# An unused tensor of 32 bytes behind the constants of an attention + mixture-of-experts kernel

## The reference, cut to what matters

```python
# q, k, v: (4 batches, 8 heads, 576 positions, 64); window 64
scores = q @ k.T / 8, masked to 0 <= i - j < 64, softmax, @ v   -> x: (2304, 512)
# mixture of experts, E = 8, hidden 1024
noisy = x @ w_gate + log1p(exp(x @ w_noise)) * noise
top2 of noisy per token, softmax over the two
out[token] += weight * (relu(x[token] @ w1[e]) @ w2[e])          # its two experts
# dense layer, hidden 2048
h = x @ w_in;  g = h if h >= 1, 0 if h <= -1, else (h + 1)**2 / 4
return g @ w_out
```

## Time and profile before

| | |
|---|---|
| runs | 1139.37, 1140.97, 1141.70 us; median 1140.97 us |
| profiled execution | 1140.15 us, span 1138.6 us from first to last instruction |
| mean granted TensorE clock | 0.976 of full speed |
| PE busy | 1086.2 us, 95% of the span |
| PEld, DVE, ACT, POOL busy | 928.5, 346.6, 351.7, 355.0 us |
| DMA | 121.96 MB, mean 107 GB/s |
| chain that ended last | PE 81%, DMA 8%, POOL 7% |

### The profile page before, as it was taken

How to read it: one execution, slowest core, us unless ns; L and a number is a source line. 1 busy time by engine, 2 the same in 40 slices (tenths; PEclk the granted TensorE clock), 3 DMA queues, 4 the chain that set the end, 5 groups by cost and what they waited for, 6 DMA issues and landing times.

```text
span 1138.6 us, 19459 instructions
## 1 busy us (share of the span) xinstructions
PE 1086.2 (95%) x6597; PEld 928.5 (82%) x6598; DVE 346.6 (30%) x652; ACT 351.7 (31%) x797; POOL 355.0 (31%) x230
## 2 busy tenths in 40 slices
PE   7999489997699999999999999999999999999998
PEld 5998368886588888888888887889889899898896
DVE  5888621221011221121122112334132242241421
ACT  4676312121121222122222212425234143252441
POOL 3000067434882917345361803750110101101000
PEclk8999689999799999999999999999999999999999
DMA  9896355778353333324141422220110101101000
GB/s 233 222 228 158 121 176 185 229 256 288 96 181 111 120 120 111 111 92 147 53 169 55 140 73 65 91 77 10 55 40 15 55 0 55 46 9 55 8 12 19
DMA packets 68706, 121.96 MB, mean 107 GB/s; under 512 B 25728, under 2 KB 30976, under 8 KB 68160
## 3 DMA queue, kind: packets, MB, share of 16 engines
q0 software_dynamic: 16688, 62.66, 17.1%
q1 hardware_dynamic: 38496, 34.72, 11.0%
q10 hardware_dynamic: 13488, 24.12, 6.5%
HBM read 87.66 MB, written 33.82 MB: 107 GB/s over the span
## 4 chain that ended last, share of the span: by engine, by line
PE 81%; DMA 8%; POOL 7%; issue 2%; DVE 1%; SPq 0%; ACT 0%; POOLq 0%; DVEq 0%
PE bank L1115 6%; PE bank L1114 6%; PE bank L1113 6%; PE bank L1053 6%; PE bank L1051 6%; PE bank L1052 6%; PE bank L1036 5%; PE bank L1038 5%; PE bank L1037 5%; PE bank L1100 5%; PE bank L1099 5%; PE bank L1098 5%; POOL Wl L378 4%; DMA x_sorted<-gath 3%; DMA gath<-x_rows,token_of 3%; PE bank L924 3%
## 5 line engine op out<-in xcount | busy, mean ns | idle before, releaser
L378 POOL TENSOR_TENSOR Wl<-stage,Wh 128x2048 fp32r<-128x2048 f32 x36 | 165.8, 4606 | 3.0
L1098 PE MATMUL bank<-zT_h,Wh 128*128 128x256 f32 x576 | 161.9, 281 | 1.0 <-DVE zT_l L861 1.0
L1099 PE MATMUL bank<-zT_l,Wh 128*128 128x256 f32 x576 | 161.8, 281 | 0.0
L1100 PE MATMUL bank<-zT_h,Wl 128*128 128x256 f32 x576 | 161.7, 281 | 0.0
L1036 PE MATMUL bank<-Wh,xT_h 128*128 x344 | 141.1, 410 | 19.7 <-POOL Wl L378 18.1
L827 DVE COPY y_out<-bank 128x512 f32<-128x512 f32 x43 | 29.7, 691 | 393.1 <-PE bank L1053 393.1
L1038 PE MATMUL bank<-Wh,xT_l 128*128 x344 | 137.4, 399 | 0.0
L1037 PE MATMUL bank<-Wl,xT_h 128*128 x344 | 136.6, 397 | 0.0
L1053 PE MATMUL bank<-Wh,hT_l 128*128 x344 | 136.4, 397 | 0.0
L1051 PE MATMUL bank<-Wh,hT_h 128*128 x344 | 135.8, 395 | 0.2 <-issue 0.2
L1052 PE MATMUL bank<-Wl,hT_h 128*128 x344 | 135.3, 393 | 0.0
(11 more groups left out here) (156 smaller groups left out, 1656.7 us busy)
## 6 DMA issues: line engine op xcount, KB each, us to landing
stage<-w POOLq DMA_DIRECT2D x32, 1024.0 KB, 5.7
x_sorted<-gath SPq DMA_DIRECT2D x43, 256.0 KB, 4.0
y_sorted<-y_out ACTq DMA_DIRECT2D x43, 256.0 KB, 2.1
x_in<-x_sorted ACTq DMA_DIRECT2D x41, 256.0 KB, 2.7
x_rows<-x_blk SPq DMA_DIRECT2D x36, 128.0 KB, 3.6
out<-o_out SPq DMA_DIRECT2D x36, 128.0 KB, 2.3
q_bd<-qT SPq DMA_DIRECT2D x16, 256.0 KB, 4.9
stage<-w_in POOLq DMA_DIRECT2D x4, 1024.0 KB, 5.7
```

The costliest lines, as they stand in the source:

```text
L378: nc.gpsimd.tensor_tensor(Wl[:, s, cols], stage[:, c % 2], Wh[:, s, cols], ALU.subtract).then_inc(w_ready, 1)
L1098: nc.tensor.matmul(here, high, zT_h[:, k], start=(k == 0), stop=False)
L1099: nc.tensor.matmul(here, high, zT_l[:, k], start=False, stop=False)
L1100: mm = nc.tensor.matmul(here, low, zT_h[:, k], start=False, stop=(k == KD - 1))
```

## The change: what it does

Behind the last of the constants one more tensor is allocated, 8 float32 values per partition, that no instruction reads or writes.

```diff
         io_t = sb("io_t", [P, 2, NT], BF16)
         io_p = sb("io_p", [P, 1])
         zeros = sb("zeros", [P, D])
+        sb("align", [P, 8])
 
 
         with ExitStack() as s1:
```

## The result

| | before | changed |
|---|---|---|
| runs, median | 1140.81 us | 1121.98 us (1121.12 to 1122.23) |
| profiled span | 1138.6 us | 1119.5 us |
| ratio | | 0.9835, 95% interval 0.9818 to 0.9852 |

The changed kernel is 18.8 us faster. The forecast was 1140.9 us, with 1138.0 to 1144.0.

What follows compares the result with a forecast made beforehand. PE was taken as busy nearly throughout the experts from 295 us and the dense layer, with DMA setting the time between 150 and 300 us. Every term was 0, bounds -12.7 and +15.7 us, giving 1140.9 us, range 1138.0 to 1144.0.

Steps and rivals of the forecast that it cites:

- rival A: Transfers of moved buffers get faster, the chip merging whole 64-byte lines; 1136.2 us at half the bound; chance 0.08.
- rival B: Transfers get slower, at the four `gath` buffers between 174 and 272 us; 1147.2 us at half the bound; chance 0.09.
- The piece of `q_bd` at the start: First 14 us, PE waits for `q_bd` after a 9.26 us piece; bounds 1.4 us less or 1.9 us more.
- the matmuls that read `id_cols`: Routing, where `id_cols` moves off the boundary: 6.1 us on the path, at most 0.6 us allowed either way.
- comparison of 104 with 86.5 ns per packet: `x_in`, `y_out` packets off the boundary took 86.5 ns; the line from `stage` packets on it gives 104 ns.
- the 1.5% more beats: Transfers of 2048 bytes take 65 beats from 32 and 66 from 64; estimated 0.8 us more on the chain.
- The term of PE's moving operands: L1098 to L1100, 1728 matmuls of 256 columns: at most 1.85 of 118.5 ns is the address; 0 taken, bound 3.2 us.
- Rival C: PE reads `zT_h` and `zT_l` faster, changing only L1098 to L1100; whole surplus gives 1137.7 us; chance 0.05.
- The term of PE's weight loads: PE loads of `Wh` on the boundary take 189 ns, `gT_h` off it 188, beside the matmuls; value 0.
- an interplay of addresses: An effect the prediction couldn't place; remaining chance 0.05, shared 0.03 faster and 0.02 slower.

Runs made afterwards that it cites:

- the pair on operands: On the kernel before, 32 unused bytes ahead of `zT_h` only: 1130.92 us; ahead of `xT_h`, `gT_h` and `zT_h`, moving the loaded stage operands but not `zT`: 1129.95 us.
- The mirrors: On the kernel before, `Wh`, `Wl` and `stage` moved 32 bytes: 1120.92 us; the same with the change's 32 bytes added: 1137.37 us.
- the one kernel made for it: Stage operands set at distances from `Wh`, `Wl` modulo 512 of `xT` 0, `hT` 16, `gT` 448, `zT` 448: 1119.37 us, one run.

## Why the prediction was wrong

The terms of everything but PE's pace held. Packets out of and into the moved buffers: 89.8 ns against 90.7, and 72.5 us on the chain against 73.1, so neither rival A nor rival B occurred. The piece of `q_bd` at the start is 9.10 us where it was 9.26, and the matmuls that read `id_cols` take 345 ns as before. ACT and DVE, `Wh` and `Wl` from `stage` and `xT_l`, and the weight loads (columns as in the earlier trace rows):

```profile
L533 ACT ACTIVATE Wh<-stage 128x512 fp32r<-128x512 f32 x16 | 10.2, 638 | 0.0
...
L819 DVE TENSOR_TENSOR xT_l<-bank,xT_h 128x512 fp32r<-128x512 f32 x43 | 29.3, 682 | 4.6 <-ACT xT_h L594 4.6
...
L1114 PEld LDWEIGHTS bank<-Wh,gT_h 128*128 128x128 f32 x288 | 54.1, 188 | 12.6 <-POOL Wl L379 1.8
```

638, 682 and 188 ns, where it was 638, 680 and 188. The prediction's comparison of 104 with 86.5 ns per packet was weaker than it looked, as single windows differ by that much. The Trainium skill's rule for transfers (DMA: Bandwidth & Descriptors, How a descriptor splits into AXI transactions), that a descriptor off a boundary of 256 bytes starts with a part transaction, is neither confirmed nor refuted: the 1.5% more beats that the prediction estimated from it can't be seen in these rows.

Two steps failed, both on PE.

1. **The term of PE's moving operands, value 0, bound 3.2 us; measured 9.2 us.** The place was right (the three lines with `zT`), the size was not. The bound took the matmul of 512 columns as purely proportional and at the best pace, since its moving operand lay on the boundary: 233.3 / 2 = 116.65 ns. But that matmul was itself slowed by the same cause. 113.4 ns is below the supposed floor, as half of 228.9 is 114.5. So a bound had been taken from a row that shared the disturbance. Rival C named this mechanism and its lines, with 1137.7 us as its price; alone it gives 1130.92 us.

2. **The term of PE's weight loads ("They also lie beside the matmuls. Value 0."); measured 10.6 us.** The comparison (189 ns on, 188 off) was right and its conclusion was not. A load keeps its duration and stays beside the matmuls, and yet its operand's address changes their pace. The second kernel of the pair on operands shows it: with only loaded operands at new distances in the expert stage and in the last matmuls of each group, 512 columns go from 233.3 to 228.9 ns. The prediction had no term for this; it is in no rival either, except for 0.03 for an interplay of addresses with "which buffers are read at the same time as `Wh`".

Behind both stands a third error. I called the old layout "a good comparison in itself, since some operands lie on multiples of 64 and others 32 past one". For PE it was blind. Each of its large matmuls pairs `Wh` or `Wl` with a stage buffer, so all of them had one operand on and one off, at the same 160 modulo 512. A comparison of rows with equal distances can't price a distance. The forecast then treated "no difference between rows" as "no cost in the rows".

The mirrors show that the distance counts and not the boundary: 1120.92 us with all operands off it, 1137.37 us with the moved ones on it. What in the chip does it is not shown. The Trainium skill (TensorE: Matmul & The Clock Gate, Step-by-step: what each phase is for) says the matrix engine has two independent read ports for the moving and the loaded operand, and that loading the next weights doesn't take read bandwidth from the running matmul. As I read it, the distance between the two should then not matter. The runs disagree: 228.9 against 233.3 ns with the loaded operand alone at new distances. That the two reads meet in the same part of the memory, at times set by the distance, is my explanation and is only argued.

Open stays what the full set of good distances is (a period of 256 fits the one kernel made for it), whether a matmul meets its own or the next load, and what puts a series into its slower rhythm at addresses that allow the faster. Also open is why the kernels with 64 unused bytes and with `Wh`, `Wl` off are 2.1 and 3.3 us faster than before: 1728 x 0.4 ns explain 0.7 us of it, and tiles 0.018 us shorter another 0.6. For the first that is within its interval (0.5 to 4.4 us). For the second (1.9 to 4.7 us) it is not; in its profile the experts' first hidden layer is ready for transposing at 160.5 us, where it was 162.5, but whether the addresses do that is not shown. And open is whether the old distance has a faster rhythm as well.

## What to carry to other kernels

Where PE is the bound, an edit that only moves buffers can change the time by 1.7%, so an effect of that size in any edit that also shifts addresses needs a control with the same edit and the addresses held. Read the start-to-start steps of long series of matmuls, not the durations of matmuls or loads, and before you price an address from rows of the same kernel, ask whether any two of those rows differ in the relation between their two operands. Small unused tensors (here 32 bytes) are a cheap trial on PE-bound code, but judge them by several runs and by the paces of all groups, since one set of addresses can have more than one steady rhythm.

## What the runs showed of the hardware that was not expected

- The same float32r matmul, with 128 x 128 loaded and its load hidden, takes 113.4 to 120.0 ns per 256 columns and 226.7 to 233.5 ns per 512, at full granted clock, depending on how far apart the two operands lie in a partition and on what precedes the series. A multiple of 64 bytes is neither needed (1120.92 us with none) nor enough (1137.37 us).
- The loaded operand's address changes the pace of the matmuls (233.3 to 228.9 ns), while the load's own duration stays at 188 ns.
- One program with fixed addresses has several steady paces: 118.2 and 113.4 ns in different groups, 12.51 and 12.20 us in neighbouring tiles. Two bf16 matmuls of 512 columns ahead of the series turn 117.8 into 113.4 ns.
